# Gate columns moved behind the last group's ranks of the attention stage

## The reference

```
k = v = pool4x4(kv) @ w_sr                       # 768 keys for a batch
x = softmax(q @ k.T / sqrt(128)) @ v             # 24576 rows of 128
# layer 0: expert = argmax(x @ w_gate)
y[i] = p_e * relu(x[i] @ w1[e]) @ w2[e]
# layer 1: expert = argmax(cosine(y, expert_emb) / tau)
out[i] = p_e * relu(y[i] @ w1b[e]) @ w2b[e]
```

## Time and profile before

| | us |
|---|---|
| median of 3 runs | 1941.06 (1939.07 to 1942.12) |
| the profiled execution | 1936.4 |
| its span | 1934.6 |
| TensorE busy | 1840.5 (95%) |
| VectorE busy | 1383.2 (71%) |
| ScalarE busy | 1236.8 (64%) |
| GpSimd busy | 791.9 (41%) |

### The profile page before, as it was taken

How to read it: one execution, slowest core, us unless ns; L and a number is a source line. 1 busy time by engine, 2 the same in 40 slices (tenths; PEclk the granted TensorE clock), 3 DMA queues, 4 the chain that set the end, 5 groups by cost and what they waited for, 6 DMA issues and landing times. The chain is left out here.

```text
span 1934.6 us, 64925 instructions
## 1 busy us (share of the span) xinstructions
PE 1840.5 (95%) x18785; PEld 1645.5 (85%) x18786; DVE 1383.2 (71%) x3563; ACT 1236.8 (64%) x2907; POOL 791.9 (41%) x1114
## 2 busy tenths in 40 slices
PE   5999999999999979999999999994999999999998
PEld 5888888888888868888888888883899999899997
DVE  2479899788888526777777777775566666666665
ACT  1367777778787636777777767663555555555554
POOL 0013333356766331445544554456233333333333
PEclk9699999999999969999999999997999999999999
DMA  7012222133444121222233211111111111111111
GB/s 278 12 49 84 90 88 68 43 105 121 129 130 121 55 76 29 68 77 70 75 75 78 47 45 45 47 41 40 44 49 49 49 49 42 45 49 49 46 49 27
DMA packets 108697, 132.17 MB, mean 68 GB/s; under 512 B 16302, under 2 KB 86074, under 8 KB 108608
## 3 DMA queue, kind: packets, MB, share of 16 engines
q1 hardware_dynamic: 78656, 83.38, 15.7%
q0 software_dynamic: 19328, 38.19, 6.0%
q10 hardware_dynamic: 10624, 9.46, 1.7%
HBM read 90.41 MB, written 42.39 MB: 69 GB/s over the span
## 5 line engine op out<-in xcount | busy, mean ns | idle before, releaser
L2143 DVE SCALAR_TENSOR_TENSOR hT_l<-ps_hidden,hT_l 128x512 f16<-128x512 f32 x412 | 282.4, 688 | 184.5 <-ACT hT_l L2100 162.6
L2100 ACT ACTIVATE hT_l<-ps_hidden 128x512 f16<-128x512 f32 x412 | 239.4, 596 | 227.8 <-PE ps_hidden L2042 224.7
L1849 DVE SCALAR_TENSOR_TENSOR hT_l<-ps_hidden,hT_l 128x512 f16<-128x512 f32 x412 | 282.0, 685 | 134.2 <-ACT hT_l L1797 115.9
L2182 POOL DMA_INDIRECT out<-out_rows_l,out_slots_l x206 | 200.0, 971 | 381.0 <-DVE out_rows_l L2151 338.0
L1797 ACT ACTIVATE hT_l<-ps_hidden 128x512 f16<-128x512 f32 x412 | 245.1, 595 | 172.1 <-PE ps_hidden L1730 113.3
L1730 PE MATMUL ps_hidden<-xT_l,W 128*128 128x256 f16 x2472 | 338.9, 274 | 1.1 <-DVE xT_l L1844 1.1
L2042 PE MATMUL ps_hidden<-xT_l,W 128*128 128x256 f16 x2472 | 338.6, 273 | 1.0 <-DVE xT_l L2129 1.0
L1744 PE MATMUL ps_y<-W,hT_l 128*128 x1648 | 307.6, 279 | 6.4 <-DVE hT_l L1849 6.4
L2056 PE MATMUL ps_y<-W,hT_l 128*128 x1648 | 293.3, 273 | 1.6 <-DVE hT_l L2143 1.6
L702 POOL DMA_INDIRECT rows<-att_rows,att_slots x192 | 189.8, 989 | 236.1 <-ACT exps L1166 97.4
L1521 POOL DMA_INDIRECT rows<-grp_rows,grp_slots x206 | 206.2, 1001 | 187.1 <-ACT grp_rows L1469 75.6
(11 more groups left out here) (223 smaller groups left out, 2909.9 us busy)
## 6 DMA issues: line engine op xcount, KB each, us to landing
x_l<-rows SPq DMA_DIRECT2D x206, 130.0 KB, 2.1
w_chunk<-in_moe_w SPq DMA_DIRECT2D x34, 512.0 KB
W<-in_kv SPq DMA_DIRECT2D x24, 512.0 KB, 8.8
q<-in_q SPq DMA_DIRECT2D x48, 256.0 KB
size_chunk<-in_moe_w SPq DMA_DIRECT2D x18, 512.0 KB
w_chunk<-in_moe_w ACTq DMA_DIRECT2D x16, 512.0 KB, 3.8
rows<-grp_rows,grp_slots POOLq DMA_INDIRECT x206
out<-out_rows_l,out_slots_l POOLq DMA_INDIRECT x206
```

The costliest lines, as they stand in the source:

```text
L1849: nc.vector.scalar_tensor_tensor(out=hT[:, p, 1, :], in0=psH[:, (HP * h + p) % HB, :], scalar=0.0, in1=hT[:, p, 0, :], op0=ALU.max, op1=AL ...
L2100: nc.scalar.activation(hT[:, p, 0, :], psH[:, p, :], ACT.Relu).then_inc(h_high, 1)
L2143: nc.vector.scalar_tensor_tensor(out=hT[:, p, 1, :], in0=psH[:, p, :], scalar=0.0, in1=hT[:, p, 0, :], op0=ALU.max, op1=ALU.subtract).then ...
```

## The change

The gate steps leave bodies 48, 49 and 51. TensorE now does steps 0 to 5 behind the whole pipeline, then the table's turn, then steps 6 to 16. ScalarE does copies 0 to 4 behind the pipeline, then its four pad fills, then copies 5 to 15 and `act_gates`. In the expert layer the wait for `gates_low` moves from before the first transpose to tile 0's first output. SyncE's loads stay where they are.

```diff
 class GateColumns:
-    UNITS = 2 * E
+    UNITS, SOON = 2 * E, 5
@@ attention, tensor
-                    if isinstance(t, int) and t == QT:
-                        if kb == 0:
-                            pe.wait_ge(exped, QT * QS)
-                        gates.pe_step(pe, kb)
-                if isinstance(t, int) and t == QT + 1:
-                    for i in range(KB, 9):
-                        gates.pe_step(pe, i)
-                if isinstance(t, int) and t == QT + 3:
-                    for i in range(9, gates.UNITS + 1):
-                        gates.pe_step(pe, i)
             pipeline(pe, body)
+            pe.wait_ge(exped, QT * QS)
+            for i in range(gates.SOON + 1):
+                gates.pe_step(pe, i)
             table.pe_turn(pe)
+            for i in range(gates.SOON + 1, gates.UNITS + 1):
+                gates.pe_step(pe, i)
@@ attention, scalar
-                    if isinstance(t, int) and t == QT:
-                        if kb == 0:
-                            act.wait_ge(q_turned, QT)
-                        gates.act_copy(act, kb)
-                if isinstance(t, int) and t == QT + 1:
-                    for i in range(KB, 9):
-                        gates.act_copy(act, i)
-                if isinstance(t, int) and t == QT + 3:
-                    for i in range(9, gates.UNITS):
-                        gates.act_copy(act, i)
-                    gates.act_gates(act)
             pipeline(act, body)
+            act.wait_ge(q_turned, QT)
+            for i in range(gates.SOON):
+                gates.act_copy(act, i)
             table.fill(act, k.region[0], range(E // 2, E), False)
+            for i in range(gates.SOON, gates.UNITS):
+                gates.act_copy(act, i)
+            gates.act_gates(act)
@@ first_experts, tensor
                 if p == 0:
                     wait(pe, added, j - 1)
+                    if isinstance(j, int) and j == 0:
+                        pe.wait_ge(gates_low, 1)
...
-            pe.wait_ge(gates_low, 1)
```

## The result

The kernel after takes 1953.32 us (1950.21 to 1954.54, 8 runs), the kernel before beside it 1940.99 (1937.15 to 1946.88, 8 runs): ratio 1.0054, 95% interval 1.004 to 1.0068, +12.3 us. The forecast was 1954.8, +13.7.

What follows compares the result with a forecast made beforehand. The prediction took the handover from attention to expert layer, at TensorE's low clock, as the place that counts: 22.05 + 0.5 more gate work, less 3.4 (ranks) and 5.4 (pads), +13.7 on 1941.1 gives 1954.8 us, range 1946 to 1959.

Steps and rivals of the forecast that it cites:

- (a): Body 48 loses gate steps 0 to 5, so group 22's ranks come 3.4 us earlier; its stall stays.
- (b): Body 49 loses steps 6 to 8; TensorE idles about 3 us before group 23's ranks; gain taken as 0.
- (c): Start of the gate phase: first product moves with GpSimd's chain, from 694.49 to 691.1.
- (d): Gate phase: all 16 products and 14 turns run at the low clock, 22.05 us more, 37.9 in all.
- (e): Table's turn between steps 5 and 6 takes TensorE 0.4 us, without a wait.
- (f): ScalarE's pads between copies 4 and 5 are hidden, 0 to 0.5 us to spare or pay; taken as 0.1.
- (g): Block end: pads leave the chain behind TensorE's last product, 6.45 us becomes 1.04, 5.4 back.
- rival C: Body 48's stall goes with the gate steps, ranks 11 us earlier: +6.1, 1947.2 us; chance 0.15 with what lies between.
- D: Group 22's ranks come no earlier, no gain in (a): +17.1, 1958.2 us; chance 0.08 for it and above.
- Rival A: Gate phase in one piece runs at full clock, 19.4 us: -2.5, 1938.6 us; chance 0.06.
- B: Clock rises halfway in the gate phase, half the steps at 1.27 us: +4 to +6, 1946 us; chance 0.06.
- (h): Expert layer 0: the moved wait for the low gate columns had 1.5 us to spare, so 0 saved.

Runs made afterwards that it cites:

- The second pair of traces: The kernels before and after, unedited, run again beside a before of 1941.0 us: after 1951.9 us, ratio 1.0055; before 1944.07 us in one run.
- pads last: Kernel after with ScalarE's four pad fills put back behind the copy of the result: 1924.78 us, ratio 1.0091 to the kernel before.
- pads early: Kernel before with only ScalarE's pads moved between copies 11 and 12 and the table's turn behind step 12: 1902.43 us, ratio 0.9971; again 1902.38 us.
- the last experiment: Pads-only kernel with copy 9 at body 50's end, copy 10 among group 23's rows, pads and table's turn one later: 1897.85 us, 0.9947 to before.
- The one kernel made to find their cause: Kernel after with SyncE's body 48 loads of w2 chunks 4 to 6 issued behind its last turn: 1920.08 us, ratio 1.0065 to before.

## Why the prediction was right

Sign, size and mechanism held. By the steps, in the distances of the two profiled executions:

| step | said | measured |
|---|---|---|
| (a) ranks of group 22 earlier | 3.4 | 18.41 - 13.72 = 4.7 |
| (b), (c) those ranks to the first product | 17.20 | 691.25 - 674.14 = 17.11 |
| (d), (e), (f) first product to the end of the last | 38.4 | 730.80 - 691.25 = 39.55 |
| (g) that end to the opening | 1.04 | 0.97 |
| sum against before | +13.7 | -4.7 - 0.1 + 23.7 - 5.5 = +13.4 |

(The third row of before is 15.85, so +23.7; the fourth 6.45.) The second pair of traces gives -5.1 + 0.0 + 22.2 - 5.5 = +11.7, and the medians gave +12.3 and +10.9, so that 13.4 comes so near to 13.7 is in part luck: in the first pair a stall of 0.9 that was priced at 0.1 and a gain in (a) that was put too low offset each other. For the change on the median, 12.3, the forecast was 1.4 too high.

(a) was sized a little small. Behind the stall it was right: from TensorE's first turn there to the ranks it is 677.29 - 669.40 = 7.89 before and 674.14 - 669.89 = 4.25 after, 3.6 less for a forecast of 3.4. The missing 1.05 lie ahead of it: that turn comes 10.52 behind the body's first before and 9.47 after. In all it is 4.7 in the first pair of traces, 5.1 in the second (18.77 - 13.72), and 3.8 to 4.0 on the chip without stalls (pads last against pads early, 7.54 and 11.57 us from first turn to ranks, give the 4.0). The stall stayed, as taken, and rival C, in which it goes with the gate steps, is contradicted by both traces of after, with 5.47 and 6.06 us of TensorE waiting in body 48. So is D.

(b) TensorE idled for 3.52 us before group 23's ranks, 3 were said; nothing came of it, since GpSimd's last send of group 22, at 688.01, still set ScalarE's last row. That the first product waits for this last row was taken as given in (c); the last experiment shows it to be a matter of the order on ScalarE, which the change left as it was.

(d) was right in the price and in the condition, 2.45 us a step and 0.50 for all of it, but one of its two reasons was wrong. I argued from TensorE's idle time ahead of the phase, "which is how it fell before", and from the long stretch at 0.50 in the earlier trace rows. The clock falls without that idle time: in the trace of the moved wait ahead of it, in the one with two copies among the rows with none since the mixes. The run with the matmuls ahead shows the steps fall back to the low clock from a full one, so the second reason is the one that holds. What it is in these steps (fp32, transposes, eight columns) that leaves the clock low, no run separates. The Trainium skill ("TensorE: Matmul & The Clock Gate", Part 1) has sustained matmul activity release the throttle. The trace of after does not agree for these matmuls: TensorE was busy for all 25.66 us from 705.14 on, at 0.50. With three 512-column matmuls added in each step it was at 1.00. Rival A, which rested on that rule, and B are out. (A's turning point was given as 1.6 us a step; with the pads no longer hidden at such a pace, as A itself has it, the same sum gives about 1.5.)

(e) the table's turn is 703.17 - 702.79 = 0.38, said 0.4, and it waited for nothing. (f) From turn 6 to product 5 it is 0.86 where no pads stand between (pads last, 690.49 - 689.63), 1.97 in the first trace of after and 1.06 in the second. So the pads cost 1.1 and 0.2; 0.1 was said with 0.5 as the upper end, and a wait of more than 1 us as a sign of being wrong (the row's idle time is 0.90). In the first trace copy 4 started 0.9 late, which no row explains, and there was no slack for it. Where pads are hidden by a hair, the cost is that of the execution one happens to look at.

(g) 5.5 back for 5.4. Taking it out (pads last) brought 4.5 of loss and taking it alone (pads early) 3.6 to 5.4 of gain. (h) 0, as the run with the wait alone shows, and rival E is out.

What stays open is the stalls marked "remote". They are in every trace taken where before runs at 1941 us, though not always in the same rows, and in none where it runs at 1907.5. The one kernel made to find their cause ran on the faster chip.

## What to carry to other kernels

Filler work was worth most between and right behind the dense matmuls: there it ran at their full clock, and in a heap of its own the same step cost 2.45 us in place of 1.27. Before moving such work behind a wait, ask what clock it will have there, not only whether the engine is free. And look at what ends the block first: here 5.4 us hung on four DMA issues that stood last in one queue, and some 4.5 more on copies queued behind rows they did not need; neither called for moving a gate step.

## What the hardware did that I had not expected

- The same kernel took 1907.5 us on one chip and 1941 on another, 1.8% apart, with a spread of at most 0.6% on each. Stalls of 2.4 to 6.4 us put down to "remote", in body 48 and at VectorE's L764, are a small part of it: the distance is 57.9 against 51.2. Expert layer 0 alone, from its first to its last transpose of `x`, took 594.9 us (719.7 to 1314.6) in the trace of before and 580.0 (706.6 to 1286.6) in that with the moved wait.
- A full clock was lost in gate steps with TensorE busy throughout: at once behind 20 matmuls and a short wait (0.86 on average from 677.36 to 680.45, 0.50 after), later behind the mixes of body 49 (still 1.00 from 671.39 to 676.78 with two copies among the rows, 0.50 from 678.32).
- Three added matmuls a step made the step shorter, 1.93 us against 2.45, at a clock that stayed full; one, at a clock that was already low, made it longer, 2.88.
